# Level products in spans of 32 tokens, and another order of the opening, in a linear attention kernel with two MLPs

## What is computed

```python
def _attn_ref(r, k, v, w, u):                      # [B=4, H=8, S=768, D=48]
    state = zeros(B, H, D, D)
    for t in range(S):
        kt, vt, rt, wt = (k[:, :, t], v[:, :, t], r[:, :, t], w[:, :, t])
        cur = einsum('bhd,bhe->bhde', u[None] * kt, vt)
        y[:, :, t] = einsum('bhd,bhde->bhe', rt, state + cur)
        state = wt[:, :, :, None] * state + einsum('bhd,bhe->bhde', kt, vt)
...
x = y by token, [3072, 384]
h = x @ w_in; g = h * clip(h + 3, 0, 6) / 6; x = g @ w_out          # w_in [384, 2048]
a = x @ w1; b = x @ w2; out = (a * b @ w3) @ w_out2                 # w1, w2 [384, 1024]
```

## Time and profile before

| | |
|---|---|
| median of 3 runs | 967.52 us (963.72 to 967.79) |
| profiled execution | 968.75 us |
| its span | 966.9 us |
| TensorE busy | 931.7 us, 96% |
| VectorE busy | 559.8 us, 58% |
| ScalarE busy | 305.9 us, 32% |
| GpSimd busy | 249.1 us, 26% |

### The profile page before, as it was taken

One profiled execution on the slowest core, in us unless ns is written; L12 is line 12 of the kernel. 1 busy time (PEld: TensorE's weight loads), 2 busy tenths in 40 slices (PEclk: granted clock), 3 DMA queues, 4 the chain that ended last, 5 costly groups with the idle time before them and its releaser, 6 DMA issues.

```text
span 966.9 us, 19789 instructions
## 1 busy us (share of the span) xinstructions
PE 931.7 (96%) x8432; PEld 848.1 (88%) x8432; DVE 559.8 (58%) x745; ACT 305.9 (32%) x508; POOL 249.1 (26%) x209
## 2 busy tenths in 40 slices
PE   3879899999999999999999999999999999999998
PEld 3556889999999999999999999998888888888887
DVE  4976877778777878777878773354323222223221
ACT  0314333333333333324242434353222222222222
POOL 0680534444444444443544310000000000000000
PEclk9979999999999999999999999999999999999999
DMA  9957343434343434342525210253010100100000
GB/s 305 348 181 243 82 132 99 125 99 124 98 125 97 126 96 127 98 125 76 148 79 144 76 33 21 80 158 104 1 65 1 52 15 30 36 5 30 1 34 33
DMA packets 62310, 93.09 MB, mean 96 GB/s; under 512 B 7895, under 2 KB 48430, under 8 KB 62094
## 3 DMA queue, kind: packets, MB, share of 16 engines
q1 hardware_dynamic: 59230, 88.16, 30.1%
q10 hardware_dynamic: 2992, 3.67, 1.3%
HBM read 76.07 MB, written 11.01 MB: 90 GB/s over the span
## 4 chain that ended last, share of the span: by engine, by line
PE 86%; DVE 6%; issue 3%; DMA 2%; POOL 1%; ACT 1%; SPq 0%; ACTq 0%; DVEq 0%
PE ps_acc L1053 11%; PE ps_acc L1054 10%; PE ps_acc L1055 10%; PE ps_h L1055 9%; PE ps_h L1054 9%; PE ps_h L1053 9%; PE ps_lv L1089 7%; PE ps_lv L1054 3%; PE ps_lv L1055 3%; PE ps_lv L1053 3%; PE ps_h L1205 3%; PE ps_acc L1125 2%; PE ps_acc L1133 2%; DVE k_sb L788 2%; DVE r_sb L788 1%
## 5 line engine op out<-in xcount | busy, mean ns | idle before, releaser
L567 ACT ACTIVATE g_hi<-gated 128x512 fp32r<-128x512 f32 x144 | 90.8, 631 | 415.7 <-DVE gated L957 293.8
L524 POOL TENSOR_TENSOR tok_a<-tok_a 128x384 f32<-128x384 f32 x126 | 156.8, 1270 | 246.1 <-DMA tok_a<-in_k 246.1
L1053 PE MATMUL ps_acc<-g_hi,w_out_hi 128*128 128x256 f32 x576 | 172.4, 299 | 0.7 <-DVE g_lo L965 0.7
L1054 PE MATMUL ps_acc<-g_hi,w_out_lo 128*128 128x256 f32 x576 | 163.9, 284 | 0.0
L1055 PE MATMUL ps_acc<-g_lo,w_out_hi 128*128 128x256 f32 x576 | 163.5, 284 | 0.0
L1053 PE MATMUL ps_h<-x_hi,w_in_hi 128*128 128x256 f32 x576 | 162.3, 282 | 0.0
L1054 PE MATMUL ps_h<-x_hi,w_in_lo 128*128 128x256 f32 x576 | 162.1, 281 | 0.0
L1055 PE MATMUL ps_h<-x_lo,w_in_hi 128*128 128x256 f32 x576 | 162.0, 281 | 0.0
L1035 DVE TENSOR_TENSOR gated<-gated,ps_lv 128x512 f32<-128x512 f32 x48 | 33.0, 688 | 186.2 <-PE ps_lv L1055 186.2
L965 DVE TENSOR_TENSOR g_lo<-gated,g_hi 128x512 fp32r<-128x512 f32 x96 | 83.5, 869 | 88.7 <-ACT g_hi L567 88.7
L1053 PEld LDWEIGHTS ps_acc<-g_hi,w_out_hi 128*128 128x128 f32 x576 | 110.4, 192 | 6.7 <-issue 2.0
(11 more groups left out here) (91 smaller groups left out, 1575.5 us busy)
## 6 DMA issues: line engine op xcount, KB each, us to landing
tok_a<-in_r SPq DMA_DIRECT2D x21, 768.0 KB, 4.5
tok_a<-in_w SPq DMA_DIRECT2D x21, 384.0 KB, 4.8
v_sb<-in_v SPq DMA_DIRECT2D x12, 384.0 KB, 3.7
x_scratch<-x_out SPq DMA_DIRECT2D x12, 384.0 KB, 4.1
x_in<-x_scratch SPq DMA_DIRECT2D x6, 768.0 KB, 6.1
tok_a<-in_k SPq DMA_DIRECT2D x22, 192.0 KB, 5.1
w3T_sb<-in_w3T SPq DMA_DIRECT2D x2, 2048.0 KB, 13.9
out<-x_out SPq DMA_DIRECT2D x5, 768.0 KB, 4.0
```

Source lines behind the costliest of these rows:

```text
L524: return nc.gpsimd.tensor_tensor(dst, x, y, ALU.mult)
L567: return nc.scalar.activation(dst, src, ACT.Copy, **scale)
L1053: nc.tensor.matmul(psum, hi, moving_hi, start=start, stop=False)
L1054: nc.tensor.matmul(psum, lo, moving_hi, start=False, stop=False)
```

## The change

Levels of 4, 8 and 16 tokens are now cut into spans of 32 tokens: four products for each head block, with 28, 24 or 16 stationary columns and 16 moving ones, each written to its own 32 partitions. Blocks of these levels do not cross a span, so nothing wanted is left out. The level of 64 is two products of 32 stationary columns; that of 32 stays. In group 1, levels 1 and 3 use two banks of `ps_acc`, and levels 1 to 3 no longer wait for the merge directly before. `keep_busy` multiplies zeros at the very start and after the first level. In the opening, scalings stand ahead of band sums and masks, weight splits and w34 parts stand elsewhere, and SP moves x before it waits for the third band sum.

```diff
+SPAN = 32
         def banks_of(p, step):
+            if p == 1 and step in (1, 3):
+                return ps_acc[:, 0:2, :]
...
             load_w_over(2)
-            load_tok_over(4)
             move_x(0)
             move_x(1)
-            load_weight(6)
-            load_weight(7)
             load_v_over(1)
             load_rk_over(2)
-            for q in range(8, 12):
+            load_tok_over(4)
+            for q in range(6, 12):
                 load_weight(q)
...
+            nc.vector.memset(y_sb[0][:], 0.0).then_inc(y_zeroed, 1)
             scale(0, 0)
             scale(0, 1)
+            scale(0, 2)
             dve.wait_ge(masks_loaded, 16 * 2)
...
+                elif p == 1 and step == 1:
+                    pe.wait_ge(state_new, updates(1))
+                elif p == 1 and step in (2, 3):
+                    pe.wait_ge(merged[1], level(1, step - 2))
                 elif step > 0:
                     pe.wait_ge(merged[p % 2], level(p, step - 1))
...
-                count = C - size
+                span = max(SPAN, 2 * size)
...
+                            for s0 in range(0, C, span):
+                                at_col, s = first + s0 // 2, cols.start + s0
+                                of_r = halves(r_g[rows, s:s + span], size)[:, :, 1, :]
+                                count = min(span - size, P // 4) if size >= P // 4 else span - size
+                                for i in range(0, span - size, count):
                                     last = nc.tensor.matmul(
+                                        psum[s0 + i:s0 + i + count, h, at_col:at_col + span // 2]
+                                        .rearrange("s (n l) -> s n l", l=size),
+                                        k_g[rows, s + i:s + i + count], of_r,
                                         start=True, stop=True, skip_group_check=True)
...
+            def keep_busy(banks):
+                for psum in banks:
+                    nc.tensor.matmul(psum, y_sb[0][:, 0, :], flat(y_sb[0]), start=True, stop=True)
+            pe.wait_ge(y_zeroed, 1)
+            keep_busy([ps_acc[:, i, :] for i in range(KT + 1)] + [ps_lv[:, i, :] for i in range(2)]
+                      + 4 * [ps_h[0][:]])
             attention(0, 0)
+            keep_busy(2 * [ps_h[0][:]])
             attention(0, 1)
```

More of the change, by code:

```diff
@@ L34 @@
 MASKED = 2
-APART = 3
+SPAN = 32
 PREPS = 7
@@ L996, in _ @@
             scale(1, 1)
-            sum_bands(2)
+            split_weight(0)
             scale(1, 2)
@@ L1002, in _ @@
             merge(1, 1)
+            sum_bands(2)
+            split_weight(2)
+            scale(1, 4)
+            split_weight(3)
             sum_bands(3)
-            scale(1, 4)
-            split_weight(2)
             split_x(0)
             split_x(1)
-            split_weight(3)
+            split_weight(4)
+            scale(1, 5)
             start(2)
             start(3)
+            split_weight(5)
             sum_bands(4)
-            scale(1, 5)
-            for q in range(4, 10):
+            for q in range(6, 10):
                 split_weight(q)
@@ L1073, in level_products @@
                 k_g, r_g, psum = flat(k_sb[p % 2]), flat(r_sb[p % 2]), banks_of(p, step)
-                count = C - size
+                span = max(SPAN, 2 * size)
                 for c in range(2):
                     for a in range(PAIRS):
-                        cols = cols_of(p, c, a)
+                        cols, first = cols_of(p, c, a), (c * PAIRS + a) * C // 2
                         for h in range(2):
                             rows = slice(h * HB, h * HB + D)
-                            first = (c * PAIRS + a) * C // 2
-                            if step == APART:
-                                for s0 in range(0, C, 2 * size):
-                                    at_col, s = first + s0 // 2, cols.start + s0
+                            for s0 in range(0, C, span):
[3 more added lines that the diff above has]
+                                for i in range(0, span - size, count):
                                     last = nc.tensor.matmul(
-                                        psum[s0:s0 + size, h, at_col:at_col + size],
-                                        k_g[rows, s:s + size], r_g[rows, s + size:s + 2 * size],
+                                        psum[s0 + i:s0 + i + count, h, at_col:at_col + span // 2]
+                                        .rearrange("s (n l) -> s n l", l=size),
+                                        k_g[rows, s + i:s + i + count], of_r,
                                         start=True, stop=True, skip_group_check=True)
-                                continue
-                            last = nc.tensor.matmul(
-                                psum[0:count, h, first:first + C // 2]
-                                .rearrange("s (n l) -> s n l", l=size),
-                                k_g[rows, cols.start:cols.start + count],
-                                halves(r_g[rows, cols], size)[:, :, 1, :], start=True, stop=True)
                 last.then_inc(products[p % 2], 1)
@@ L1228, in _ @@
             form_w34(3, 1)
+            form_w34(4, 0)
             attention(1, 2)
-            form_w34(4, 0)
+            form_w34(4, 1)
+            form_w34(5, 0)
             attention(1, 3)
-            form_w34(4, 1)
-            for f in (5, 6, 7):
+            form_w34(5, 1)
+            for f in (6, 7):
                 form_w34(f, 0)
```

41 lines of the change are left out of this document (20 added, 21 removed).

## The result

The changed kernel takes 972.75 us (median of 12 runs, 970.36 to 977.2); the kernel before, beside it, 967.84 (12 runs, 963.72 to 970.92). The ratio is 1.0054, 95% interval 1.0039 to 1.0069: half a per cent slower, where 941.0 was forecast. The profiled execution took 972.78, its span is 971.0.

The account below looks back on a forecast made before the run. TensorE, busy 931.7 of 966.9 us, was taken as the bound, with idle or slow time before the first hidden product. 968.75 less 16.8 (levels) and 11 (opening) gave 940.95, so 941 us; range 930 to 954.

Parts of the forecast that it names:

- Size of a level: TensorE's levels of 4, 8 and 16: each new burst 1.1 us, saving 2.1 us a group.
- Rival 1: Level products: a small product costs a record's time however few its columns; 1047 us at 34 ns, chance 0.05.
- both rules: TensorE's small matmuls: about 60 cycles of overhead each, and a floor of about 25 ns between starts.
- The level of 64: TensorE's level of 64 as 64 records: 1.08 us, nothing changes; bounds 0.69 and 2.15.
- How much reaches the end: Ten groups' level bursts: shorter ones count only where VectorE waited for them; 16.8 us in sum.
- The factors for the levels of 4 and 8: Savings counted over ten groups: level of 4 nine times (7.0 us), half that of 8 ten times (3.6).
- Rival 2: VectorE keeps the gain: levels of 4 and 8 free nothing, its scalings being at half speed beside GpSimd; 951.5, chance 0.15.
- Its mark for being right: TensorE's waits for VectorE's merges exceed 15 us.
- The opening: Before the first hidden product: it starts at 78 instead of 92.12, 14 us earlier, of which 11 us count.
- scaling 6: A VectorE scaling in the opening, worked out to be done at 31 us.
- Rival 3: The opening gains nothing: zeros delay the first level, and loads or GpSimd's products set the pace; 952, chance 0.13.
- Rival 5: Whole kernel: the parts cancel or the levels cost what they did, so no change; chance 0.02.

Follow-up runs that it names:

- nozeros32: The changed kernel without its twelve products of zeros, VectorE zeroing the banks instead: 958.5 us, ratio 0.989 to the kernel before.
- light64: span64 with GpSimd's products by token cut to 24 of 384 columns from the fifth chunk on (work left out): 921.9 us, ratio 0.9523.
- span64: The changed kernel with levels of 4, 8 and 16 in spans of 64 tokens, 64 records a level instead of 128: 947.05 us, ratio 0.9773.
- open64: The changed kernel with 64-token spans in the opening and 32-token spans in all slots: 969.1 us, ratio 1.0027.
- lightopen64: span64 with GpSimd's products by token cut to 24 of 384 columns for the opening's three chunks (work left out): 942.3 us, ratio 0.9759.
- late64: span64 with the slots' products of the levels of 8 and 16 behind the projection instead of ahead of it: 934.0 us, ratio 0.9644.

## Why the prediction was wrong, step by step

- **Size of a level.** 1.1 us with bounds 1.0 to 1.38 was forecast; from start to next row the three levels are 1.28 to 1.51, 1.16 to 1.34 and 1.15 to 1.35. The step holds near its upper bound, which single bursts of the level of 4 pass: 1.63 us a group instead of 2.1. Rival 1 fell, and so did both rules that the prediction took from the Trainium skill (TensorEngine Tiling (Array Packing), Instruction Overhead; TensorE: Matmul & The Clock Gate, Wait — 56ns, not 53.3ns?): a record costs 9 to 12 ns, not 25. The level of 64 changed nothing, as said.
- **How much reaches the end (the step that failed, first part).** 16.8 us were forecast and the slots got 3.1 us slower, though the bursts saved 16.3. The sum asked what other engines do with a shorter burst and never whether TensorE can be fed with 256 instructions in 1.2 us: the supply of instructions stood at nothing in it, without a reason. Stops took 5.4 us and the clock behind one of them 3.4. That the stops cost this is shown by nozeros32, where a shift by 48 instructions removes all of them from the slots, brings the half clock from 125 us on down from 20.4 to 13.7 us, and wins 14.3 us, 3.8 of them in the opening.
- **VectorE's share (second part).** The factors for the levels of 4 and 8 were read from waits of the old kernel. Rival 2 was right in its kind: waits for merges rose by 6.9 us, the half clock behind two of them cost 3.4 more, and where bursts are shorter still, the waits came to 17.5. Its mechanism, scalings at half speed beside GpSimd, is shown by light64. Its mark for being right, over 15 us, was missed by the changed kernel and met by span64.
- **The opening (the step that failed, second part).** The first hidden product was to come 14 us earlier, with 11 us left at the end; it came 0.4 later. Two causes, each removed by itself: the stops cost 7.3 us (92.5 to 85.25 in open64), and VectorE beside GpSimd 8.8 (85.3 to 76.5 in lightopen64, where 78 was forecast for the changed kernel). The working had the third and fourth level at 20 and 23.6; they began at 22.83 and 32.37, each after a stop in the level before, and scaling 6, "done at 31", ended at 43.5 (at 35.4 in span64, without stops). GpSimd's part was measured on top of span64, where group 1's first scaling ran at half speed; in the changed kernel that scaling came later and ran at full speed, so how much GpSimd costs there isn't shown. Rival 3 ("the opening gains nothing") was right about the first hidden product, and in span64 also in blaming GpSimd's products. The zeros, which it blamed too, cost nothing with spans of 64; with spans of 32 they do harm, but by their number and not by the delay.
- **The forecast that the parts add up.** They don't: 0.9905 and 0.9972 alone, 1.0054 together. The opening's twelve products of zeros move every later burst by 48 records against the blocks. Without them (nozeros32) both parts together give 0.989, which is about the product of the two. Rival 5, the parts cancel, had been given 0.02; it is the one nearest to what was measured.

What stays open: why a packet that could begin 299 records ahead often begins much later, down to the border itself; and the share of the clock alone, which no run could hold fixed.

## What to carry to other kernels

Before cutting matmuls into more, smaller ones, count instructions by time. Here TensorE went on 2.3 to 2.9 us after a packet of 256 of its instructions had begun, and no packet began more than 299 records ahead; a burst that uses 256 in 1.2 us may stop, and whether it does depends on its place in the whole program. Look for TensorE rows that wait by "issue" in the middle of a burst; halving the records (spans of 64 here) or moving the count by a few instructions tells at once whether they are of this kind. And where a wait is lifted by shorter work, look who was just in time before: the engine behind it (here VectorE beside GpSimd) is the next bound, and an order that gives it time can be worth much (13 us in late64, 8 in the kernel before).

## What was not expected of the hardware

- TensorE's instructions come in 16 KB packets of 256; at every 256th it can stand still, for 0.4 to 5.3 us in these runs, and goes on 2.3 to 2.9 us after the packet began.
- Nine 8-column products at the start of a program of 12,000 matmul records cost 24 us, and twelve 512-column ones left out win 14, both with spans of 32; with spans of 64 the same twelve left out win nothing.
- 128 records with 16 moving columns last longer (1.15 to 1.5 us) than 64 with 32 (0.85 to 1.01), for the same result.
